# Unread products of a constant table between the steps of a threshold search (greedy routing of a mixture of experts)

## The chip, the cores and the metric

The program runs on one core of a Trainium2 chip. The metric is the device time of one execution in microseconds (us). The engines named here are TensorE (PE; PEld is its weight load), VectorE (DVE), ScalarE (ACT), GpSimd (POOL) and the DMA queues.

## The reference

Three layers follow one another on 20,224 tokens of 256 features: a gated recurrence, a mixture of 8 experts with greedy routing under a capacity, and a mixture of 8 experts with the best expert for each token. The change touches the routing of the second layer alone.

```python
# layer 1: h = f * h + (1 - f) * x, over 4 sequences of 5056 tokens, f from a sigmoid
# layer 2: greedy routing, cap = N // E = 2528 tokens to an expert
logits = x @ w_gate
order = np.argsort(-logits.flatten())
for idx in order:
    tok, e = (int(idx) // E, int(idx) % E)
    if assigned[tok] >= 0 or counts[e] >= cap:
        continue
    assigned[tok] = e
    counts[e] += 1
for e in range(E):
    mask = assigned == e
    out[mask] = np.maximum(x[mask] @ w1[e], 0.0) @ w2[e]
# layer 3: argmax expert for each token, result scaled by its softmax weight
```

## The kernel before

The kernel has six stages with a barrier between them: constants, the recurrence with the scores (`scan_stage`), greedy routing (`route_greedy`), the experts of layer 2, the routing of layer 3 and its experts.

Scores lie in a table of 128 partitions x 8 experts x 160 columns. Greedy routing is done in 7 phases (`PH`). In a phase each unassigned token bids for its best open expert (`bids`, lines 747 to 758, all on DVE), and a search finds the lowest threshold at which no expert overflows. A search round tests 16 thresholds at once. DVE compares all bids with them (`above`, line 787) in 4 pieces (`PIECES`). PE counts, for each expert and threshold, the bids above: 20 products of `choice` (64 wide weights) with 128 columns of `above`, 5 to a piece, added up in `cP` (line 681). DVE takes the diagonal and sums it (`part_cnt`, lines 794 and 796), PE sums over groups (`eP`, line 685), DVE compares with what each expert needs (`fills`, line 798), PE adds over experts (`aP`, line 687), and DVE counts (`nfill`, line 800) and makes the next thresholds (lines 805 and 808). Every step waits for the one before through a semaphore; only the pieces of `above` overlap with PE.

A phase has 3 rounds (`TRIED`) and then a test whether all bids above the low end fit (line 695). Only where they don't are 4 more rounds and an exact cut run. In these inputs one phase of seven does that, so there are 6 x 3 + 7 = 25 rounds.

After the last phase `place_rows` and `place_products` find for each slot of an expert the token that lies there. PE adds 160 products of 320 columns into `r_found_ps` (line 480), the first with start=True. That tensor isn't read before line 548, after all 160. `c.emin_full` is a constant bf16 table, 8 - e for expert e, made before the first stage.

Of the kernel before, what the change touches and what calls it, by code (L numbers as in the profile page):

```python
# [30 lines left out]
P = 128  # L31
# [47 lines left out]
def alone(eng, passed):  # L79

    eng.sem_inc(passed, 1)
# [357 lines left out]
def place(nc, ctx, m, cols):  # L439

    r = Consts()
    sb = lambda n, s, d=F32: ctx.enter_context(nc.sbuf_tensor(m + n, s, d))
    sem = lambda n: ctx.enter_context(nc.semaphore(m + n))
    r.cols = cols
    r.own = sb("own", [P, E])
    r.run = sb("run", [P, E, NG])
    r.shift = sb("shift", [P, E])
    r.mine = sb("mine", [P, E, NG])
    r.slot = sb("slot", [P, NG])
    r.slot_i = sb("slot_i", [P, 3, NG], I32)  # L450
    r.slot_b = sb("slot_b", [P, 2, NG], BF16)
    r.grid_col = sb("grid_col", [P, NG], BF16)


    r.hit_place = sb("hit_place", [P, 2, J // 2, P, 2], BF16)
    r.hit_tile = sb("hit_tile", [P, 2, J // 2, cols, 2], BF16)
    r.hit_row = sb("hit_row", [P, 2, J // 2, 2, cols, 2], BF16)
    r.found = sb("found", [P, 2, cols])
    r.base_ps = ctx.enter_context(nc.psum_tensor(m + "base_ps", [P, 2, E], F32))
    r.found_ps = ctx.enter_context(nc.psum_tensor(m + "found_ps", [P, 2, cols], F32))  # L460
    r.own_ready = sem("p_own_ready")
    r.base_ready = sem("p_base_ready")
    r.tile_ready = sem("p_tile_ready")
    r.part_ready = sem("p_part_ready")
    r.hits_ready = sem("p_hits_ready")
    r.hits_used = sem("p_hits_used")
    return r


def place_products(pe, c, r):  # L470

    pe.wait_ge(r.own_ready, 1)
    pe.matmul(r.base_ps[:, 0, :], c.tri[:], r.own[:], start=True, stop=True)
    pe.matmul(r.base_ps[:, 1, :], c.ones[:], r.own[:], start=True, stop=True).then_inc(r.base_ready, 1)

    def group(g, b, begin, end):
        pe.wait_ge(r.hits_ready, g + 1)
        pe.wait_ge(r.part_ready, g + 1)
        for j in range(J):
            mm = pe.matmul(r.found_ps[:], r.hit_place[:, b, j // 2, :, j % 2], r.hit_row[:, b, j // 2, :, :, j % 2],  # L480
                           start=(begin and j == 0), stop=(end and j == J - 1), skip_group_check=True)
        mm.then_inc(r.hits_used, 1)

    group(0, 0, True, False)
    group(1, 1, False, False)
    with pe.Fori(1, NG // J // 2 - 1) as g:
        group(2 * g, 0, False, False)
        group(2 * g + 1, 1, False, False)
    group(NG // J - 2, 0, False, False)
    group(NG // J - 1, 1, False, True)  # L490
# [60 lines left out]
def route_greedy(nc, c, w1, w2):  # L551
# [3 lines left out]
    with ExitStack() as ctx:  # L555
# [59 lines left out]
        r = place(nc, ctx, "r_", NG)  # L615
# [25 lines left out]
        @block.sync  # L641
        def _(sp):
            load_weights(sp, c, w1, w2, 0, raw)
# [13 lines left out]
        @block.tensor  # L657
        def _(pe):
            groups = NG // Q
            piece = groups // PIECES  # L660

            def columns(q):
                return choice[:, q, :, :].rearrange("p e n -> p (e n)")

            def count_mask(n, mask):

                pe.wait_ge(mask_ready, n + 1)
                for q in range(groups):
                    mm = pe.matmul(qP[:], columns(q), mask[:, q * Q:(q + 1) * Q], start=(q == 0), stop=(q == groups - 1))
                mm.then_inc(mask_counted, 1)  # L670

            def sum_mask(n):
                pe.wait_ge(mask_row_ready, n + 1)
                pe.matmul(nP[:], c.ones[0:E * Q, :], mask_row[:], start=True, stop=True).then_inc(mask_summed, 1)

            def count_round(n):
                for q in range(groups):
                    if q % piece == 0:
                        pe.wait_ge(above_ready, PIECES * n + 1 + q // piece)

                    mm = pe.matmul(cP[:].rearrange("m t q -> m (t q)"), columns(q),  # L681
                                   above[:, :, q * Q:(q + 1) * Q], start=(q == 0), stop=(q == groups - 1))
                mm.then_inc(counted, 1)
                pe.wait_ge(part_ready, n + 1)
                pe.matmul(eP[:], c.sel[:], part_cnt[:], start=True, stop=True).then_inc(summed, 1)
                pe.wait_ge(fills_ready, n + 1)
                pe.matmul(aP[:], c.ones_b[:], fills[0:E, :], start=True, stop=True).then_inc(filled, 1)

            with pe.Fori(0, PH) as k:
                pe.wait_ge(choice_ready, k + 1)  # L690
                alone(pe, passed)
                for n in range(TRIED):
                    count_round(k * ROUNDS + n)
                pe.wait_ge(try_ready, k + 1)
                pe.matmul(nP[:], c.ones[0:E, :], cnt_row[:], start=True, stop=True).then_inc(tried_summed, 1)
                pe.wait_ge(over_ready, k + 1)
                alone(pe, passed)
                over_now = pe.value_load(over[0:1, 0:1], min_val=0, max_val=1)
                with pe.If(over_now > 0):
                    for n in range(TRIED, ROUNDS):  # L700
                        count_round(k * ROUNDS + n)
                    count_mask(2 * k, sure)
                    sum_mask(2 * k)
                    pe.wait_ge(own_edge_ready, k + 1)
                    pe.matmul(oP[:], c.tri[:], own_edge[:], start=True, stop=True).then_inc(before, 1)
                    count_mask(2 * k + 1, taken)
                    sum_mask(2 * k + 1)
                with pe.If(over_now < 1):

                    for sem_of_round in (counted, summed, filled):  # L710
                        pe.sem_inc(sem_of_round, ROUNDS - TRIED)
                    pe.sem_inc(before, 1)
                    pe.sem_inc(mask_counted, 2)
                    pe.sem_inc(mask_summed, 2)
            place_products(pe, c, r)
# [992 lines left out]
```

## Time and profile before

| | us |
|---|---|
| median of 3 runs | 2828.97 |
| lowest, highest | 2825.3, 2830.41 |
| profiled execution, its own time | 2830.13 |
| span of its trace | 2828.4 |
| search, first and last product of `cP` (start) | 255.2, 522.6 |
| products of `r_found_ps` (start) | 554.3 to 595.3 |

PE is busy for 87% of the span, DVE for 45%. That is an average over stages: in the experts PE is the busy engine, in the search it is DVE, and PE's products are short stations of a chain between two DVE instructions. How to read the views: a wait names the instruction for which an engine sat idle, and a timeline row gives start, duration, instruction and the idle time before it in brackets.

### The profile page before, as it was taken

To read this page: it belongs to the slowest core of one execution; us is meant where nothing else is said; L and a number is where in the kernel's file an instruction comes from. 1 tells how busy PE (TensorE), PEld (TensorE's weight loads), DVE (VectorE), ACT (ScalarE), POOL (GpSimd) and SP (SyncE) were. 2 spreads that over 40 slices of the span, in tenths; PEclk is the share of its full clock that TensorE was granted. 3 is DMA by queue.
4 is the path that set the end of the run, shared out by engine and by line. 5 is a ranking of instruction groups with operands and counts; after the bars stand their busy time and mean duration, and the time that the engine had idled before them with its cause. 6 is when DMAs were issued, how large, how long until landed. Compare 5 with 4: busy or idle time off the path is not lost. (4 is left out here: it accounts for less than half of the span.)

```text
span 2828.4 us, 42796 instructions
## 1 busy us (share of the span) xinstructions
PE 2450.3 (87%) x14391; PEld 2092.6 (74%) x14392; DVE 1277.1 (45%) x2306; ACT 738.9 (26%) x1386; POOL 797.8 (28%) x765
## 2 busy tenths in 40 slices
PE   7992333269999999999999945999999999999998
PEld 6991222148888888888888832888888888888887
DVE  6776777863434343434433367333333333333332
ACT  3540000132222222222222214222222222222222
POOL 2332000031313131322311120435535443535332
PEclk9995555589999999999999978999999999999999
DMA  7991000021212121212111111212212121211111
GB/s 245 311 305 49 0 0 0 0 64 55 75 37 74 37 72 39 67 45 68 44 37 45 37 52 38 67 45 68 70 45 72 44 74 45 69 45 40 39 45 34
DMA packets 100823, 183.66 MB, mean 65 GB/s; under 512 B 12797, under 2 KB 70399, under 8 KB 100800
## 3 DMA queue, kind: packets, MB, share of 16 engines
q1 hardware_dynamic: 33328, 75.00, 8.2%
q0 software_dynamic: 24960, 66.02, 7.9%
q10 hardware_dynamic: 42512, 42.38, 4.3%
q8 instruction: 9, 0.15, 0.0%
q14 instruction: 14, 0.11, 0.0%
HBM read 120.26 MB, written 65.44 MB: 66 GB/s over the span
## 5 line engine op out<-in xcount | busy, mean ns | idle before, releaser
L1639 DVE SCALAR_TENSOR_TENSOR m_hl<-m_hP,m_hh 128x512 fp32r<-128x512 f32 x352 | 243.5, 692 | 664.4 <-ACT m_hh L1596 664.4
L1331 DVE SCALAR_TENSOR_TENSOR m_hl<-m_hP,m_hh 128x512 fp32r<-128x512 f32 x320 | 221.4, 692 | 581.3 <-ACT m_hh L1284 581.3
L1596 ACT ACTIVATE m_hh<-m_hP 128x512 fp32r<-128x512 f32 x352 | 210.5, 598 | 664.3 <-PE m_hP L1548 664.3
L1284 ACT ACTIVATE m_hh<-m_hP 128x512 fp32r<-128x512 f32 x320 | 191.1, 597 | 680.9 <-PE m_hP L1192 680.9
L1104 POOL COPY m_idx<-rows_i 128x4 int32 (+1 forms) x41 | 7.6, 185 | 1049.8 <-PE m_tP L1161 703.6
L681 PE MATMUL cP<-above,choice 128*64 128x128 bf16 x500 | 73.7, 314 | 156.0 <-DVE above L787 156.0
L1490 POOL DMA_INDIRECT m_xg<-y_rows,m_idx x180 | 173.8, 965 | 86.2 <-POOL m_idx L1486 39.3
L1501 POOL DMA_INDIRECT out_dram<-m_rows,m_dest x176 | 175.5, 997 | 69.6 <-issue 52.5
L681 PEld LDWEIGHTS cP<-above,choice 128*64 128x64 bf16 x500 | 50.1, 162 | 175.9 <-DVE above L787 175.9
L1108 POOL DMA_INDIRECT m_xg<-h_rows,m_idx x164 | 156.4, 954 | 74.1 <-issue 40.8
L1486 POOL COPY m_idx<-rows_i 128x4 int32 (+1 forms) x45 | 8.4, 187 | 526.4 <-PE m_tP L1538 459.6
L1559 PEld LDWEIGHTS m_yP<-w_1h,m_hh 128*128 128x128 f32 x704 | 103.9, 189 | 19.9 <-DVE m_hl L1639 9.8
L1559 PEld LDWEIGHTS m_yP<-w_0h,m_hh 128*128 128x128 f32 x704 | 103.9, 189 | 19.6 <-DVE m_hl L1639 9.5
L1559 PE MATMUL m_yP<-w_1h,m_hh 128*128 128x256 f32 x704 | 117.9, 290 | 0.2
L499 ACT ACTIVATE r_hit_row<-r_hit_tile,part 128x1280 bf16<-128x1280 bf16 x20 | 27.2, 1362 | 347.7 <-DVE r_hit_tile L535 347.7
L1559 PE MATMUL m_yP<-w_0h,m_hh 128*128 128x256 f32 x704 | 117.9, 290 | 0.2
L1548 PE MATMUL m_hP<-m_xh,w_0h 128*128 128x512 f32 x352 | 112.2, 400 | 2.2 <-DVE m_xl L1635 1.4
L1559 PE MATMUL m_yP<-w_1h,m_hl 128*128 128x256 f32 x704 | 113.0, 282 | 0.0
L1559 PE MATMUL m_yP<-w_0h,m_hl 128*128 128x256 f32 x704 | 112.9, 282 | 0.0
L1559 PE MATMUL m_yP<-w_0l,m_hh 128*128 128x256 f32 x704 | 112.1, 281 | 0.0
L1559 PE MATMUL m_yP<-w_1l,m_hh 128*128 128x256 f32 x704 | 112.1, 281 | 0.0
L1548 PE MATMUL m_hP<-m_xh,w_1h 128*128 128x512 f32 x352 | 111.4, 398 | 0.0
(300 smaller groups left out, 5582.7 us busy)
## 6 DMA issues: line engine op xcount, KB each, us to landing
w_raw<-in_moe_w_dram SPq DMA_DIRECT2D x32, 1024.0 KB, 6.9
y_rows<-m_rows ACTq DMA_DIRECT2D x41, 516.0 KB, 3.5
f_in<-in_f_logit_dram SPq DMA_DIRECT2D x39, 512.0 KB, 4.6
x_in<-in_x_dram SPq DMA_DIRECT2D x39, 512.0 KB, 6.9
h_rows<-rows ACTq DMA_DIRECT2D x39, 512.0 KB, 5.7
m_xg<-y_rows,m_idx POOLq DMA_INDIRECT x180
out_dram<-m_rows,m_dest POOLq DMA_INDIRECT x176
m_xg<-h_rows,m_idx POOLq DMA_INDIRECT x164, 2.8
```

The lines of the kernel that those rows point to most:

```text
L499: act.activation(r.hit_row[:, b, :, 0, :, :].rearrange("p g n j -> p g (n j)"), r.hit_tile[:, b, :, :, :].rearrange("p g n j -> p g (n j)" ...
L681: mm = pe.matmul(cP[:].rearrange("m t q -> m (t q)"), columns(q), above[:, :, q * Q:(q + 1) * Q], start=(q == 0), stop=(q == groups - 1))
L1108: pool.indirect_dma_start(xg[:, k, :], None, src[:, :], bass.IndirectOffsetOnAxis(ap=idx[:, k:k + 1].bitcast(U32), axis=0)).then_inc(gathe ...
L1284: act.activation(hh[f % 2][:], hP[f % 2][:], ACT.Relu).then_inc(hh_ready, 1)
L1331: dve.scalar_tensor_tensor(out=hl[f % 2][:], in0=hP[f % 2][:], scalar=0.0, in1=hh[f % 2][:].bitcast(F32), op0=ALU.max, op1=ALU.subtract).t ...
L1486: pool.tensor_copy(idx[:], c.rows_i[:, bass.ds(i * TPC, TPC)]).then_inc(idx_ready, 1)
L1490: pool.indirect_dma_start(xg[:, k, :], None, src[:, :], bass.IndirectOffsetOnAxis(ap=idx[:, k:k + 1].bitcast(U32), axis=0)).then_inc(gathe ...
L1501: pool.indirect_dma_start(dst[:, :], bass.IndirectOffsetOnAxis(ap=dest[:, k:k + 1].bitcast(U32), axis=0), rows[:, k, :], None, bounds_chec ...
L1548: mm = pe.matmul(hP[f % 2][:], c.w1_s[b][s][:, d, f * P:(f + 1) * P], x[:, d, :], start=(q == 0), stop=(q == len(terms) - 1))
L1559: mm = pe.matmul(yP[k][:, 0:D], h[f % 2][:, k * P:(k + 1) * P], c.w2_s[b][s][:, f, :], start=(f == 0 and q == 0), stop=(f == FC - 1 and q ...
L1596: act.activation(hh[f % 2][:], hP[f % 2][:], ACT.Relu).then_inc(hh_ready, 1)
L1639: dve.scalar_tensor_tensor(out=hl[f % 2][:], in0=hP[f % 2][:], scalar=0.0, in1=hh[f % 2][:].bitcast(F32), op0=ALU.max, op1=ALU.subtract).t ...
```

## The change

In `route_greedy` the PE program gets a helper that issues n products of `c.emin_full` into `r.found_ps` (128 wide weights, 320 columns, bf16). Each is a group of its own, and nobody reads it. The helper is called before the waits of pieces 2, 3 and 4, before the wait for `part_cnt`, before the wait for `fills`, and three times after `aP`: 8 products in each round, 200 in 25 rounds. No semaphore, no other engine and no other stage is touched.

```diff
+            def keep_going(n):
+
+                for _ in range(n):
+                    pe.matmul(r.found_ps[:], c.emin_full[:, 0, 0:P], c.emin_full[:, 0:2, :],
+                              start=True, stop=True, skip_group_check=True)
+
             def count_round(n):
                 for q in range(groups):
                     if q % piece == 0:
+                        if q:
+                            keep_going(1)
                         pe.wait_ge(above_ready, PIECES * n + 1 + q // piece)
 
                     mm = pe.matmul(cP[:].rearrange("m t q -> m (t q)"), columns(q),
                                    above[:, :, q * Q:(q + 1) * Q], start=(q == 0), stop=(q == groups - 1))
                 mm.then_inc(counted, 1)
+                keep_going(1)
                 pe.wait_ge(part_ready, n + 1)
                 pe.matmul(eP[:], c.sel[:], part_cnt[:], start=True, stop=True).then_inc(summed, 1)
+                keep_going(1)
                 pe.wait_ge(fills_ready, n + 1)
                 pe.matmul(aP[:], c.ones_b[:], fills[0:E, :], start=True, stop=True).then_inc(filled, 1)
+                keep_going(3)
```

On PE, in the loop over phases, the end of a search round stands like this before (the last two pieces, the two sums, and the first piece of the next round):

```order
L681 MATMUL cP<-above,choice 64x128 [waits r_above_ready]
L681 MATMUL cP<-above,choice 64x128 x4
L679 REGISTER_ALU
L681 MATMUL cP<-above,choice 64x128 [waits r_above_ready]
L681 MATMUL cP<-above,choice 64x128 x4
L684 REGISTER_ALU
L685 MATMUL eP<-part_cnt,sel 128x16 [waits r_part_ready]
L687 MATMUL aP<-fills,ones_b 128x16 [waits r_fills_ready]
L679 ISA
L681 MATMUL cP<-above,choice 64x128 [waits r_above_ready]
```

The same place on PE after the change:

```order
L689 MATMUL cP<-above,choice 64x128 x4
L679 MATMUL r_found_ps<-emin_full 128x320
L687 REGISTER_ALU
L689 MATMUL cP<-above,choice 64x128 [waits r_above_ready]
L689 MATMUL cP<-above,choice 64x128 x4
L679 MATMUL r_found_ps<-emin_full 128x320
L693 REGISTER_ALU
L694 MATMUL eP<-part_cnt,sel 128x16 [waits r_part_ready]
L679 MATMUL r_found_ps<-emin_full 128x320
L697 MATMUL aP<-fills,ones_b 128x16 [waits r_fills_ready]
L679 MATMUL r_found_ps<-emin_full 128x320 x3
L687 ISA
```

Every added product stands ahead of the product that waits, never behind it, and the order of the others is as it was.

## Rows read from the trace of the kernel before

**Rows 1.** The page: span, and the granted clock in 40 slices.

```profile
span 2828.4 us, 42796 instructions
...
PEclk9995555589999999999999978999999999999999
```

**Rows 2.** Who waited for whom, 255 to 538 us: total, times, longest.

```profile
PE cP L681 <- DVE above L787: 156.0, 25, 36.2
...
DVE part_q L794 <- PE cP L681: 17.5, 25, 0.8
DVE fills L798 <- PE eP L685: 17.4, 25, 0.7
...
DVE any_fills L800 <- PE aP L687: 7.1, 25, 0.3
```

**Rows 3.** Timeline around one round: start, duration, instruction, idle time before.

```profile
506.95 2.95 PE L681 MATMUL cP<-above,choice 128*64 128x128 bf16 x20 [14.75 <-DVE above L787]
...
509.94 0.28 DVE L794 TENSOR_TENSOR part_q<-cP,diag 64x128 f32<-64x128 f32 x1 [0.36 <-PE cP L681]
...
512.60 3.03 DVE L787 TENSOR_TENSOR above<-bid,thr 128x640 bf16<-128x640 f32 x4
...
513.48 2.95 PE L681 MATMUL cP<-above,choice 128*64 128x128 bf16 x20 [1.77 <-DVE above L787]
514.21 0.50 PEld L681 LDWEIGHTS cP<-above,choice 128*64 128x64 bf16 x5 [0.24 <-DVE above L787]
...
515.68 0.50 PEld L681 LDWEIGHTS cP<-above,choice 128*64 128x64 bf16 x5 [0.23 <-DVE above L787]
516.46 0.28 DVE L794 TENSOR_TENSOR part_q<-cP,diag 64x128 f32<-64x128 f32 x1 [0.83 <-PE cP L681]
...
517.11 0.60 PE L685 MATMUL eP<-part_cnt,sel 64*128 64x16 f32 x2 [0.69 <-DVE part_cnt L796]
...
518.04 0.19 PE L687 MATMUL aP<-fills,ones_b 8*128 8x16 bf16 x1 [0.33 <-DVE fills L798]
...
519.12 3.03 DVE L787 TENSOR_TENSOR above<-bid,thr 128x640 bf16<-128x640 f32 x4
```

**Rows 4.** Timeline, PE alone, 554 to 557.5 us.

```profile
554.26 3.55 PE L480 MATMUL r_found_ps<-r_hit_row,r_hit_place 128*128 128x320 bf16 x13 [11.04 <-ACT r_hit_row L499]
```

**Rows 5.** Timeline, PE alone, 558.5 to 577 us.

```profile
561.16 1.29 PE L480 MATMUL r_found_ps<-r_hit_row,r_hit_place 128*128 128x320 bf16 x8 [0.71 <-ACT r_hit_row L499]
563.31 1.29 PE L480 MATMUL r_found_ps<-r_hit_row,r_hit_place 128*128 128x320 bf16 x8 [0.86 <-ACT r_hit_row L499]
```

**Rows 6.** Line 480, 552 to 557.5 us: durations ns (min, median, max).

```profile
L480 PEld LDWEIGHTS r_found_ps<-r_hit_row,r_hit_place x14: 103/144/145, 554.2 to 557.4; 128*128 128x128 bf16 x14
L480 PE MATMUL r_found_ps<-r_hit_row,r_hit_place x13: 396/468/469, 554.3 to 557.4; 128*128 128x320 bf16 x13
```

**Rows 7.** Line 480, 560 to 594 us.

```profile
L480 PE MATMUL r_found_ps<-r_hit_row,r_hit_place x132: 300/302/305, 559.7 to 593.3; 128*128 128x320 bf16 x132
```

**Rows 8.** Line 681.

```profile
L681 PE MATMUL cP<-above,choice x500: 310/314/317, 255.2 to 522.6; 128*64 128x128 bf16 x167
```

**Rows 9.** Line 685.

```profile
L685 PE MATMUL eP<-part_cnt,sel x50: 370/380/394, 258.9 to 523.9; 64*128 64x16 f32 x50
```

**Rows 10.** Line 1181, 700 to 1600 us.

```profile
L1181 PE MATMUL m_sP<-m_wg,m_yT x550: 175/256/257, 699.8 to 1584.5; 128*128 128x8 f32 x184
```

**Rows 11.** Busy time of each engine by stretch, then granted clock, DMA.

```profile
255.00:538.00 283.00, 101.92 (x635) 72.19 (x635) 209.73 (x549) 0.00 (x0) 0.00 (x0) 0.50 0.00 0
563.00:595.00 32.00, 19.99 (x125) 11.11 (x126) 31.12 (x46) 20.60 (x16) 0.00 (x0) 1.00 0.00 0
164.00:168.00 4.00, 3.35 (x30) 3.03 (x28) 3.22 (x6) 1.69 (x4) 1.86 (x2) 1.00 0.93 316
168.00:169.00 1.00, 1.00 (x9) 1.00 (x8) 1.00 (x2) 0.60 (x1) 0.00 (x0) 0.74 1.08 371
```

**Rows 12.** Timeline, PE alone, 164 to 173 us.

```profile
165.09 1.85 PE L259 MATMUL sP<-wg,h 128*128 128x8 f32 x16
167.54 0.65 PE L237 MATMUL fP<-ident,f_in 128*128 128x128 f32 x4 [0.60 <-DMA x_in<-in_x_dram]
```

## The prediction

> **What bounds the kernel now.** I read the page first for the clock by slices: TensorE is granted half speed (1.2 GHz) in the slices of the greedy search and full speed (2.4 GHz) nearly everywhere else [rows 1]. The table by stretch says the same for 255 to 538 us: clock 0.50, PE busy 102 of 283 us, DVE 210 [rows 11]. So the search belongs to DVE, and PE matters only where DVE waits for it. The waits give these: 17.5 us for `cP`, 17.4 for `eP`, 7.1 for `aP`, in 25 rounds each, 42 us of the search in all [rows 2]. All else in a round is DVE's own work. The timeline of one round shows the stations, from `above` at 512.60 to the next at 519.12, 6.52 us: DVE waits 0.83, 0.70 and 0.28 us [rows 2, 3]. PE also waits: 1.77 us ahead of the first piece, 0.69 and 0.33 ahead of the sums, and 14.75 us ahead of a phase, while DVE makes the bids [rows 3]. The added products go into these gaps, except the long one.
>
> The change can act in two ways only: through time that an added product takes from one that DVE waits for, and through the granted clock.
>
> **The price of an added product at 1.2 GHz.** The same shape (320 columns, 128 wide weights) runs in line 480. In the stretch at 1.2 GHz 13 of them take 3.55 us, the last 0.47, so they start every (3.55 - 0.47)/12 = 0.26 us [rows 4, 6]; at 2.4 GHz 8 take 1.29, one 0.30, so every 0.141 us [rows 5, 7].
>
> Between pieces: pieces start every (515.68 - 513.48)/3 = 0.733 us, as DVE delivers them [rows 3]. The last one runs from 515.68 to 516.43 (513.48 + 2.95), 0.75 us for five products of 0.314, so one starts every (0.75 - 0.314)/4 = 0.109 us [rows 3, 8]. A piece then occupies PE for 0.545 us, and with an added product for 0.81, which is 0.07 to 0.08 more than DVE's pace. Three insertions push the last piece back by 0.22 us, and DVE waits for it. 25 rounds: 5.5 us. At 2.4 GHz a piece takes 5 x 0.056 + 0.141 = 0.42 us and nothing is late.
>
> The other five cost nothing. The one behind `cP` ends 0.3 us into a gap of 0.69; the one behind `eP` has 0.33 us of gap for 0.26, and its results drain beside the wait; the three behind `aP` need 0.8 of 1.77 us [rows 3]. If the middle one didn't fit, `aP` would be at most 0.14 us late. The three ahead of the overflow test end before it, since DVE has four small instructions to do first. Queue and semaphores are as before. `r_found_ps` is written first for real with start=True, after a long DVE stretch.
>
> Weights: the filler has 128 wide ones, and those of `choice` come back behind it. In line 480 each product loads such weights (0.144 us) and they still start every 0.26 us, so they are hidden [rows 4, 6]. I take nothing for them; the other bound is one load of 0.144 exposed at each insertion, 3 x 25 x 0.144 = 10.8 us.
>
> The Trainium skill, TensorE: Matmul & The Clock Gate, section "The mechanism" of Part 3, speaks against the change: a weight load overlaps products in flight only where it goes to other rows of the array. By that rule both swaps would show, and twice the bound above would be added. The row of 13 products at a pace of 0.26 us doesn't bear it out.
>
> **What the clock would give.** At 2.4 GHz the last piece ends earlier by 4 x (0.109 - 0.056) plus some 0.09 on the last product (320 columns: 0.468 against 0.302, of which the columns are 0.12), 0.30 us. `eP` is two products, 0.60 us together; a product of the same kind with 8 columns takes 0.256 at 2.4 GHz against 0.380, so 0.60 x 0.256/0.380 = 0.40, 0.20 us less [rows 3, 9, 10]. `aP`, 0.19, loses perhaps 0.03. Sum 0.53 us for a round that is wholly at 2.4 GHz, and it doesn't pay the 0.22. Even the first round of a phase, where DVE waits only 0.36 us for `cP` because it has other work, can take the 0.30 [rows 3]. Upper bound of the change: 25 x 0.53 = 13.3 us.
>
> **Does the clock rise, and where.** Set the density of each stretch beside its clock. The search before streams 20 x 128 = 2,560 columns in 6.52 us, 390 a us, and stays at 1.2 GHz throughout [rows 3, 11]. Line 480 started from a long idle time, streamed without a gap at 1.2 GHz, and was at 2.4 GHz soon after 557.5 us; it stays there at 8 x 320 columns every 2.15 us, 1,190 a us [rows 4, 5, 11]. After the change a round has two halves. From the first piece to the end of the filler behind `cP` PE streams 3,840 columns in some 3.2 us (1.2 GHz: nearly without a gap, like line 480). The rest, some 3.5 us, has four fillers and two small sums, 1,280 columns, under 400 a us: as thin as the search before. The nearest row at 2.4 GHz for a thin stretch lies in the recurrence: PE looks busy for 3.35 of 4 us at 164 to 168, but much of it is 16 products of 8 columns (165.09) and then 0.60 us of idle time; right behind it the clock falls (0.74 in 168 to 169) [rows 11, 12]. So I expect that the dense half raises the clock in part of the rounds, and that the thin half loses it before the next dense one: the clock is up where little is to be gained. Where it rises near the end of the dense half, `eP` and `aP` become 0.23 us shorter, sometimes with a part of the last piece. I take 0.25 us in 10 of 25 rounds, between none and all by nothing better than the split of the round: 2.5 us back.
>
> Sum: 5.5 - 2.5 = 3.0 us. The profiled execution took 2830.13 (1.2 above the median of the three runs), so 2833.1 in its terms and 2832.0 against the median. All differences below 0.2% (5.7 us) can't be told from none by a measurement of this kernel.
>
> **The rivals.**
> - The clock holds at 2.4 GHz from the first burst of a phase to its last round. For it: PE's gaps within a round shrink to under 1 us, and line 480 holds 2.4 GHz while PE is busy for 20 of 32 us [rows 11]. Against it: the thin half. Time: the first round of each phase stays slow (7 x 0.22 = 1.5 us), 18 others gain 0.53 (9.5): -8 us, 2821.
> - The skill's page on TensorE, section "Why this matters for your kernels", ties the fall to idle gaps between bursts alone. By it this rival would win. The fall at 168 us, behind a gap of 0.60 us, speaks against it.
> - Slower: the weight swaps show. At an insertion one load of 0.144 us comes on top, each piece starts 0.22 instead of 0.07 us late, and the end of `cP` moves by 0.66 us a round: +16.4 - 2.5 = +13.9, 2843. For it: `cP` changes from 64 to 128 wide weights and back, which no row shows. Against it: the pace of line 480. It decides from 0.036 us exposed at an insertion (2.7 us over 75 of them, on top of 3.0).
> - The clock never rises: +5.5, 2834.5, within my forecast's range.
> - Between the first two: 2.4 GHz is held through some phases, by how they fall; -5 to 0 us.
>
> **How the numbers follow.** Forecast (with the clock never up) 0.52, clock held 0.22, weight swaps 0.14, in between 0.12. The likeliest time is 2832.0, its own range 2829 to 2836. To leave out no more than 2 in 10 the range takes in most of the held clock (to 2820) and the lighter part of the exposed loads (to 2839). Faster by over 0.2%: most of the held clock, 0.19. Slower: the swaps and the edge of the forecast, 0.19. The same: 0.62.
>
> **What would show it.** In the trace after: the granted clock alternates between 0.50 and 1.00 in the search; the pieces of `cP` start 0.8 us apart in rounds at 1.2 GHz, 0.73 in those at 2.4; DVE's wait for `cP` grows from 17.5 us towards 20 and those for `eP` and `aP` shrink by 1 to 3 us in all. I am wrong if the clock is 1.00 through whole phases (DVE's three waits then lose 8 us or more), or if the pieces start over 0.85 us apart. The placing of tokens, the experts and the time outside 255 to 538 us stay as they are.

## The result and the profile after

| | before | after |
|---|---|---|
| median of 6 runs, us | 2826.59 | 2849.32 |
| lowest to highest | 2825.08 to 2830.41 | 2843.87 to 2853.62 |
| ratio | | 1.0075 (1.0065 to 1.0085) |
| profiled execution, span | 2828.4 | 2845.8 |

The kernel became slower by 0.75%, 21 us (18 to 24; the two medians lie 22.7 us apart). The forecast was 2832.0, with a range from 2820 to 2839.

The page after, where the clock by slices reads as before [rows 1]:

```profile
span 2845.8 us, 43196 instructions
...
PEclk9995555589999999999999978999999999999999
```

The waits around the search, 249 to 545 us (total, times, longest), to be read beside [rows 2]:

```profile
PE cP L689 <- DVE above L798: 141.4, 25, 34.8
DVE part_q L805 <- PE cP L689: 40.7, 25, 1.8
...
DVE fills L809 <- PE eP L694: 15.9, 25, 0.7
...
DVE any_fills L811 <- PE aP L697: 7.0, 25, 0.3
```

DVE waits 40.7 us for `cP` where it waited 17.5; for `eP` 15.9 instead of 17.4 and for `aP` 7.0 instead of 7.1. The sum is 63.6 against 42.0: 21.6 us more, which is as much as the result. The span of this execution is only 17.4 us longer because its recurrence, which runs ahead of the changed code, ended some 5 us sooner than in the execution before (the first product of the search starts at 250.3 instead of 255.2).

The timeline of PE for one round at 1.2 GHz (start, duration, instruction, idle time before), to be read beside [rows 3]:

```profile
520.73 0.74 PE L689 MATMUL cP<-above,choice 128*64 128x128 bf16 x5 [14.76 <-DVE above L798]
521.41 0.45 PE L679 MATMUL r_found_ps<-emin_full 128*128 128x320 bf16 x1
521.78 0.74 PE L689 MATMUL cP<-above,choice 128*64 128x128 bf16 x5
...
525.32 0.60 PE L694 MATMUL eP<-part_cnt,sel 64*128 64x16 f32 x2 [0.31 <-DVE part_cnt L807]
525.86 0.45 PE L679 MATMUL r_found_ps<-emin_full 128*128 128x320 bf16 x1
526.25 0.19 PE L697 MATMUL aP<-fills,ones_b 8*128 8x16 bf16 x1
526.38 0.98 PE L679 MATMUL r_found_ps<-emin_full 128*128 128x320 bf16 x3
528.22 0.74 PE L689 MATMUL cP<-above,choice 128*64 128x128 bf16 x5 [0.86 <-DVE above L798]
```

Pieces start 1.05 us apart (520.73, 521.78), not 0.733 as before and not 0.81 as forecast. The filler starts 0.68 us after its piece, though five products at 0.109 occupy 0.545, and the next piece starts 0.37 us after the filler, though 320 columns occupy 0.26. So 0.13 us is lost ahead of the filler and 0.11 behind it, and no semaphore is named for either.

The clock did in kind what was forecast. Busy time by stretch, then the granted clock:

```profile
415.00:421.00 6.00, 5.14 (x28) 2.70 (x27) 3.95 (x9) 0.00 (x0) 0.00 (x0) 0.50 0.00 0
422.00:424.00 2.00, 1.10 (x7) 0.47 (x6) 1.41 (x6) 0.00 (x0) 0.00 (x0) 1.00 0.00 0
425.00:428.00 3.00, 3.00 (x18) 1.71 (x17) 1.60 (x3) 0.00 (x0) 0.00 (x0) 0.50 0.00 0
```

The dense half of a round (to 421) runs at 1.2 GHz, the thin one (422 to 424) at 2.4, and the next dense one at 1.2 again. In the whole search 7 such stretches had the full clock, 24 us together. In the thin stretch `eP` is down to 0.39 us:

```profile
421.78 0.39 PE L694 MATMUL eP<-part_cnt,sel 64*128 64x16 f32 x2 [0.30 <-DVE part_cnt L807]
```

### The profile page after: what moved, and what is told of

Its sections match the earlier page's. It is cut to its first block and busy times, and to the rows that moved or that the text cites. A ratio compares the mean times of both kernels' runs of the same rounds, so it can differ in the third digit from the quotient of the medians.

```text
span 2845.8 us, 43196 instructions
## 1 busy us (share of the span) xinstructions
PE 2504.4 (88%) x14591; PEld 2104.0 (74%) x14592; DVE 1277.2 (45%) x2306; ACT 738.3 (26%) x1386; POOL 798.8 (28%) x765
## 5 line engine op out<-in xcount | busy, mean ns | idle before, releaser
L1119 POOL DMA_INDIRECT m_xg<-h_rows,m_idx x164 | 156.4, 954 | 74.1 <-issue 40.7
L1559 PE MATMUL m_hP<-m_xl,w_0h 128*128 128x512 f32 x352 | 111.3, 398 | 0.0
```

Source lines behind the costliest of these rows:

```text
L1119: pool.indirect_dma_start(xg[:, k, :], None, src[:, :], bass.IndirectOffsetOnAxis(ap=idx[:, k:k + 1].bitcast(U32), axis=0)).then_inc(gathe ...
L1559: mm = pe.matmul(hP[f % 2][:], c.w1_s[b][s][:, d, f * P:(f + 1) * P], x[:, d, :], start=(q == 0), stop=(q == len(terms) - 1))
```

## The experiments

All times are against the kernel before on the same chip in the same session. The chips differed: before had a median of 2875.96 us beside the first four kernels, 2830.87 beside the next four, and 2830.09 beside the last two. Only differences are compared. A round's length is read from the starts of `above` on DVE in each trace.

### Fillers as wide as their neighbours (e1_narrow)

```diff
-                    pe.matmul(r.found_ps[:], c.emin_full[:, 0, 0:P], c.emin_full[:, 0:2, :],
+                    pe.matmul(r.found_ps[0:E * Q], c.emin_full[:, 0, 0:E * Q], c.emin_full[:, 0:2, :],
```

> The fillers get 64 wide weights, as cP has, and write 64 partitions; columns, number and places stay. Theory W (the trace after shows pieces 1.055 us apart where 0.545 + 0.267 were expected: 0.24 us is lost at each insertion because the weights change between 64 and 128 wide, and such a load does not overlap the product in flight): pieces at 1.2 GHz start 0.81 us apart, a round takes 6.75 instead of 7.48 us, time +1 to +5 us against before. Rival S (any foreign product loses this time, by its other PSUM bank, its own start, or the semaphore of the load behind it): pieces stay 1.05 us apart, time +19 to +24 us.

The edit is against the kernel after. Measured: ratio 1.0004 (0.9995 to 1.0013), +1 us. A round at 1.2 GHz takes 6.73 us. PE's timeline of the first two pieces of a round:

```profile
508.99 0.74 PE L689 MATMUL cP<-above,choice 128*64 128x128 bf16 x5 [14.76 <-DVE above L798]
509.53 0.47 PE L679 MATMUL r_found_ps<-emin_full 128*64 128x320 bf16 x1
509.79 0.74 PE L689 MATMUL cP<-above,choice 128*64 128x128 bf16 x5
```

The filler starts 0.54 us after its piece and the next piece 0.26 after the filler: both pauses are gone and 0.80 is left, as the columns alone give. Same place, same columns, same tensor, same semaphores; only the width of the weights (and with it the partitions of the output) is another. S is out. Width of weights and partitions of the output change together in all runs here, so they aren't told apart.

The weight loads show where the time goes. After the change, the load of the first filler and that of the piece behind it:

```profile
521.40 0.10 PEld L679 LDWEIGHTS r_found_ps<-emin_full 128*128 128x128 bf16 x1 [0.17 <-issue]
...
521.78 0.50 PEld L689 LDWEIGHTS cP<-above,choice 128*64 128x64 bf16 x5 [0.28 <-issue]
```

The same two with 64 wide fillers:

```profile
509.42 0.18 PEld L679 LDWEIGHTS r_found_ps<-emin_full 128*64 128x64 bf16 x1
...
509.73 0.56 PEld L689 LDWEIGHTS cP<-above,choice 128*64 128x64 bf16 x5
```

With equal widths a load starts 0.11 and 0.06 us ahead of its product (509.53, 509.79), while the product before still runs. With unequal widths it starts with its product (521.41, 521.78), and the idle time before it has no releaser but "issue".

The time of this kernel isn't a measure of the width alone: its rounds at 1.2 GHz are 0.75 us shorter than after (7.48), 19 us in 25 rounds, and its search is at full clock for 41 us instead of 24. The added columns cost it some 5 us (25 x 0.20), of which the clock gives most back.

### No fillers between the pieces (e2_none_between)

```diff
-                        if q:
-                            keep_going(1)
```

> The three fillers between the pieces of a round are left out, the five others stay. If all the loss is at the insertions between pieces, a round takes 6.53 us or less, and the time is that of before or 0 to 3 us less (the clock may still rise in some rounds). If the fillers behind cP, eP and aP cost something too (the middle one stands in the shortest gap), the time is above before by up to 25 x 0.14 = 3.5 us.

The edit is against the kernel after. Measured: ratio 0.9999 (0.9990 to 1.0009), no difference. Rounds take 6.53 us, the clock stays at 1.2 GHz, and the waits are those of [rows 2]:

```profile
DVE part_q L803 <- PE cP L687: 17.5, 25, 0.8
DVE fills L807 <- PE eP L692: 17.5, 25, 0.7
```

The five fillers behind `cP`, `eP` and `aP` cost nothing that shows in DVE's waits, though they are 128 wide as well: what a change of width takes there falls into PE's own waits.

### Only the fillers between the pieces (e3_only_between)

```diff
                 mm.then_inc(counted, 1)
-                keep_going(1)
...
-                keep_going(1)
...
-                keep_going(3)
```

> Only the three fillers between the pieces stay (128 wide weights). If the loss is there, rounds at 1.2 GHz take 6.53 + 3 x 0.32 = 7.48 us, the clock rises in fewer rounds since five fillers are gone, and the time is +20 to +24 us. If the loss is made by the sum of all fillers (the queue, instruction fetch), it falls to 3/8 of it, +8 us.

The edit is against the kernel after. Measured: ratio 1.0085 (1.0071 to 1.0098), +24 us. Rounds at 1.2 GHz take 7.48 us, as after. The three fillers between the pieces make the whole loss. The five others in the kernel after gave back at most the difference to its +21 us, which the two intervals don't tell from nothing; in the traces its search is at full clock for 24 us, this one's for 14.

### The swap without the columns (e4_thin, e5_thin96, e9_thin64)

Three fillers in a round, between pieces, of 32 columns only, with 128, 96 and 64 wide weights; the edit is against e3_only_between. e5_thin96 and e9_thin64 ran once each and are read from their traces, not from their times.

```diff
-                    pe.matmul(r.found_ps[:], c.emin_full[:, 0, 0:P], c.emin_full[:, 0:2, :],
+                    pe.matmul(r.found_ps[:, 0, 0:32], c.emin_full[:, 0, 0:P], c.emin_full[:, 0, 0:32],
```

The other two have `r.found_ps[0:96, ...]` with `0:96` and `r.found_ps[0:64, ...]` with `0:64`.

> As the kernel with fillers only between the pieces, but of 32 columns instead of 320, with the same 128 wide weights. Theory W: a piece then takes 0.545 + 0.03 + 0.24 = 0.81 us, pieces start 0.81 apart, the last is 0.24 late, +6 us. If the loss comes from the columns (a product of 320 columns that takes longer beside DVE or in this bank) a piece takes 0.57, less than DVE's 0.733, and nothing is late: 0.

> The thin filler (32 columns, three in a round, between pieces) with 96 wide instead of 128 wide weights; cP keeps 64. If any change of width costs (theory W), pieces at 1.2 GHz start 0.81 us apart and a round takes 6.77, as with 128. If only the full 128 wide load is special (its faster kind of load), pieces start 0.735 apart, a round takes 6.53. Read from the trace, not from the time.

> Control for the thin fillers: 32 columns, three in a round between pieces, now with the 64 wide weights that cP has. Theory W (a change of width drains the array): a piece takes 0.545 + 0.03, pieces start 0.735 us apart, a round takes 6.53. If any foreign product between cP's costs: 0.81 and 6.77, as with 128 wide weights. Read from the trace.

PE's timeline from one piece to the next, 128 wide:

```profile
516.31 0.74 PE L689 MATMUL cP<-above,choice 128*64 128x128 bf16 x5 [1.77 <-DVE above L795]
516.98 0.21 PE L679 MATMUL r_found_ps<-emin_full 128*128 128x32 bf16 x1
517.12 0.74 PE L689 MATMUL cP<-above,choice 128*64 128x128 bf16 x5
```

96 wide:

```profile
515.63 0.74 PE L689 MATMUL cP<-above,choice 128*64 128x128 bf16 x5 [14.76 <-DVE above L795]
516.30 0.26 PE L679 MATMUL r_found_ps<-emin_full 128*96 128x32 bf16 x1
516.50 0.74 PE L689 MATMUL cP<-above,choice 128*64 128x128 bf16 x5
```

64 wide:

```profile
517.77 0.74 PE L689 MATMUL cP<-above,choice 128*64 128x128 bf16 x5 [1.77 <-DVE above L795]
518.31 0.23 PE L679 MATMUL r_found_ps<-emin_full 128*64 128x32 bf16 x1
518.51 0.74 PE L689 MATMUL cP<-above,choice 128*64 128x128 bf16 x5
```

| weights of the filler | piece to piece, us | round, us |
|---|---|---|
| 128 wide | 0.81 | 6.77 |
| 96 wide | 0.87 | 6.92 |
| 64 wide, like `cP` | 0.74 (DVE's pace) | 6.53 |

With 128 wide weights the time was 1.0025 (1.0016 to 1.0034), +7 us. The filler of 64 wide weights starts 0.54 us behind its piece, the two others 0.67. With 96 wide weights I had said 0.81 or 0.735; it is 0.87, so a change of width costs there too, and 0.05 us more than with 128. So the loss isn't a property of the full width but of the change, as far as fillers wider than their neighbours show it; a narrower one was not tried.

Why 96 is dearer stands in the weight loads. The filler's load, 128 wide:

```profile
516.98 0.10 PEld L679 LDWEIGHTS r_found_ps<-emin_full 128*128 128x128 bf16 x1 [0.17 <-issue]
```

96 wide:

```profile
516.30 0.16 PEld L679 LDWEIGHTS r_found_ps<-emin_full 128*96 128x96 bf16 x1 [0.17 <-issue]
```

The 96 wide load takes 0.06 us longer. Both fillers start 0.67 us behind their piece, and it is behind the filler that 96 loses: the next piece starts 0.20 us after it, not 0.14. So the part of the loss behind the filler fits the filler's own load, which nothing hides: 0.10 of the 0.11 us with 128 wide weights. The 0.13 us ahead of it are the same for both.

### Fillers sized to the gaps (e6_dense)

The edit is against the kernel after. Weights 64 wide; 1 x 192 columns between pieces, 3 x 300 behind `cP`, 1 x 300 behind `eP`, 6 x 320 behind `aP`.

```diff
+            def keep_going(n, cols=320):
+                table = c.emin_full[:].rearrange("p e n -> p (e n)")
+                spare = r.found_ps[0:E * Q].rearrange("p a n -> p (a n)")
+                for _ in range(n):
+                    pe.matmul(spare[:, 0:cols], table[:, 0:E * Q], table[:, 0:cols],
+                              start=True, stop=True, skip_group_check=True)
...
-                            keep_going(1)
+                            keep_going(1, 192)
...
-                keep_going(1)
+                keep_going(3, 300)
...
-                keep_going(1)
+                keep_going(1, 300)
...
-                keep_going(3)
+                keep_going(6)
```

> Fillers with 64 wide weights, sized to fit each gap at 1.2 GHz (1 of 192 columns between pieces, 3 of 300 behind cP, 1 of 300 behind eP, 6 of 320 behind aP). Nothing is late at 1.2 GHz, and a round has some 6,200 columns. If density is what was missing, the clock rises in the first round of a phase and holds to its last: 18 of 25 rounds take about 6.0 us instead of 6.53, time -7 to -10 us. If the clock still falls in every round: -1 to -4. If more fillers cost by themselves (queue, instruction fetch): above 0.

Measured: ratio 0.9975 (0.9963 to 0.9987), 7 us faster than before (4 to 10). DVE's three waits sum to 32.9 us in its trace, 9.1 less than before. Clock by stretch (the rounds of the first phase, the bids behind them, and the whole search):

```profile
255.00:275.00 20.00, 14.06 (x110) 9.39 (x110) 15.20 (x44) 0.00 (x0) 0.00 (x0) 0.91 0.00 0
275.00:288.00 13.00, 0.00 (x0) 0.00 (x0) 9.59 (x21) 0.00 (x0) 0.00 (x0) 0.52 0.01 3
...
255.00:514.00 259.00, 124.19 (x943) 83.47 (x944) 198.82 (x517) 0.00 (x0) 0.00 (x0) 0.74 0.00 0
```

A later round at the full clock, DVE's waits for PE:

```profile
437.60 3.03 DVE L800 TENSOR_TENSOR above<-bid,thr 128x640 bf16<-128x640 f32 x4
441.19 0.28 DVE L807 TENSOR_TENSOR part_q<-cP,diag 64x128 f32<-64x128 f32 x1 [0.56 <-PE cP L691]
...
442.27 0.23 DVE L811 TENSOR_SCALAR fills<-eP,need_p 128x16 bf16<-128x16 f32 x1 [0.48 <-PE eP L696]
442.78 0.17 DVE L813 TENSOR_SCALAR_CACHE_REDUCE any_fills<-aP 128x16 f32<-128x16 f32 x1 [0.27 <-PE aP L699]
...
443.63 3.03 DVE L800 TENSOR_TENSOR above<-bid,thr 128x640 bf16<-128x640 f32 x4
```

The round takes 6.03 us (437.60 to 443.63) instead of 6.52. DVE waits 0.56, 0.48 and 0.27 us, against 0.83, 0.70 and 0.28 [rows 2, 3]. The clock is lost in every stretch of bids (0.52) and comes back in the first round or after it, so first rounds take 6.3 to 6.5 us.

### Fillers through the bids as well (e7_through_bids, e8_wide_bids)

```diff
+            def during_bids(k):
+                for step, n, cols in ((2, 5, 300), (3, 3, 300), (4, 1, 320), (5, 1, 320), (6, 5, 300), (7, 3, 300),
+                                      (8, 1, 320), (9, 1, 320), (10, 1, 240), (11, 3, 300), (12, 4, 320)):
+                    pe.wait_ge(dv, SETUP + k * PHASE + step)
+                    keep_going(n, cols)
```

and 4 fillers each before the wait for the test and at the end of the phase without overflow. e8_wide_bids is the same with 128 wide weights.

> As the dense kernel, and fillers also beside each of DVE's steps of the bids (PE waits for the step before, then issues what fits) and around the test at the end of a phase. If the clock is held from phase to phase, all 25 rounds take 6.0 us: -11 to -14 us. If it's lost in the 3 us around the test alone: first rounds a little slower, -9 to -12. Rival: DVE's steps of the bids slow down beside PE's reads, or PE comes late into a phase: a gain smaller than that of the dense kernel.

> As the kernel with fillers through the bids, but with 128 wide weights. Theory W prices a swap at 0.11 to 0.13 us at 1.2 GHz and about 0.09 at 2.4, so at a held 2.4 GHz a piece with its filler takes 0.28 + 0.08 + 0.2 = 0.56 us, less than DVE's 0.733, and the width costs nothing: within 2 us of the 64 wide kernel. If the clock is at 1.2 when a phase begins, its first round takes 7 us or more. If the width costs time also at 2.4 GHz: +5 or more against the 64 wide kernel.

Measured: 64 wide 0.9972 (0.9961 to 0.9984), not to be told from e6_dense (0.9975); 128 wide 1.0010 (1.0002 to 1.0019). The first expectation failed. The fillers didn't hold the clock through a phase (the search as a whole, and the bids of one phase, 64 wide weights):

```profile
255.00:520.00 265.00, 188.10 (x1147) 113.40 (x1148) 202.67 (x522) 0.00 (x0) 2.86 (x1) 0.74 0.00 0
280.00:294.00 14.00, 8.76 (x34) 3.70 (x32) 10.23 (x25) 0.00 (x0) 0.00 (x0) 0.76 0.01 2
```

The mean clock of the search is 0.74, the same as without fillers in the bids, and rounds of 6.54 and 6.03 us follow one another. What the clock wins in the bids, where DVE waits for no product, it loses within the rounds: DVE's three waits sum to 35.0 us, against 32.9 in e6_dense. Why is open. The trace is that of the slowest of the six executions (2829.57 us, median 2823.38), whose search began 5.5 us later than that of e6_dense, so it stands for the clock and the rounds, not for the time.

The second failed as well in its main number (11 us above the 64 wide kernel, not within 2), since the clock wasn't held there either, but its two kinds of round answer the question. At 1.2 GHz a round takes 7.28 us. At 2.4 GHz one takes 6.03, as with 64 wide weights (starts of `above`):

```profile
296.99 3.03 DVE L812 TENSOR_TENSOR above<-bid,thr 128x640 bf16<-128x640 f32 x4
...
303.02 3.03 DVE L812 TENSOR_TENSOR above<-bid,thr 128x640 bf16<-128x640 f32 x4
```

PE in that round:

```profile
297.87 0.47 PE L692 MATMUL cP<-above,choice 128*64 128x128 bf16 x5 [0.85 <-DVE above L812]
298.27 0.26 PE L682 MATMUL r_found_ps<-emin_full 128*128 128x192 bf16 x1
298.60 0.47 PE L692 MATMUL cP<-above,choice 128*64 128x128 bf16 x5
```

Here the filler starts 0.40 us behind its piece (0.30 in e6_dense, 438.48 to 438.78), so the swap still costs 0.10, but the piece with it fits into DVE's 0.733. In this kernel the width is paid only where the clock is low.

### The dense tail alone (e10_dense_tail)

```diff
-                        if q:
-                            keep_going(1, 192)
```

> The dense kernel without its fillers between the pieces; the ten behind cP, eP and aP stay. cP's own 2,560 columns are then all that PE streams in that half of a round. If the tail's fillers are enough to hold 2.4 GHz once it is there, the time is that of the dense kernel, -6 to -9 us. If the first half is then too thin, the clock falls within rounds and little is left: -1 to -4 us.

The edit is against e6_dense. Measured: ratio 0.9981 (0.9972 to 0.9990), 5 us faster, between the two expectations. The search as a whole:

```profile
255.00:514.00 259.00, 134.10 (x850) 85.47 (x850) 196.87 (x515) 0.00 (x0) 0.00 (x0) 0.65 0.00 0
```

The mean clock is 0.65 against 0.74 with the three fillers between pieces. More rounds stay at 6.53 us, but those that are at full clock take 6.03 or 6.04. DVE's three waits sum to 35.1 us, 2.2 more than in e6_dense. The difference between the two kernels (0.0006) is within their intervals.

## Why the prediction was wrong

- **What bounds the search**: right. The whole difference is in DVE's three waits for PE; in the experts and the layer behind, the last 2,220 us of the kernel, PE is busy as long as before (2130 and 2129 us) at the same clock, 0.98.
- **The lag of the pieces**: the step that failed. I counted the columns alone, took the weights as hidden, and got 0.22 us a round. The change of width adds 0.24 us at each of three insertions, and the pieces start 1.05 us apart, beyond the 0.85 that I had named as the sign of being wrong: a round at 1.2 GHz takes 7.48 us instead of 6.53. 3 x (1.05 - 0.735) = 0.95 us, over 25 rounds 23.6; the clock gives some 2 us back and 21.6 remain. The columns' part was right: with 64 wide weights a round takes 6.73, 0.20 more.
- **Why the row misled me**: 13 products in a row each loaded new 128 wide weights at a pace of 0.26 us [rows 4]. That shows that loads hide behind products of the same width. It says nothing of a 128 wide load behind a 64 wide product, and I put the one for the other although I wrote that no row shows the change. The bound that I gave (one load of 0.144 exposed, 10.8 us) was too small too: neither the filler's load nor that of the piece behind it runs ahead, and an insertion loses 0.24 us, 75 x 0.24 = 18 us. The bound should have been two loads, 21.6 us. That 0.24 is near two loads doesn't make it two loads: the rows show 0.13 ahead of the filler's load and 0.11 behind, and what the engine does in the 0.13 is not shown.
- **The rule that I set aside**: by the Trainium skill (TensorE: Matmul & The Clock Gate, "The mechanism" in Part 3) a load overlaps products in flight only where it goes to other rows of the array. The same section also excepts a load that goes to a background buffer, which I left out. The rule called for a slower kernel, and the kernel is slower; with twice my bound, as I had worked it out, my sum would have been 24.6 us for the 21 measured. As I quoted it, it isn't borne out: in e1_narrow weights of one width on the same 128 rows are loaded 0.11 us ahead of their product, and in e1_narrow and e9_thin64 the filler follows its piece without a pause. What the runs show is a cost for a change of width.
- **The fillers behind `cP`, `eP` and `aP`**: right, they cost nothing (e2_none_between).
- **What the clock gives**: right. `eP` 0.39 us at 2.4 GHz (0.40 forecast), a wholly fast round 6.03 (6.52 - 0.53 = 5.99 forecast).
- **Where the clock rises**: right in kind. 7 short stretches, mostly in the thin half, 24 us in all, and no phase at full clock. By the sum above it is worth about 2 us (2.5 forecast). The rounds say the same: from the first `above` to the last the search takes 285.4 us instead of 264.8, 20.6 more, where 24 rounds wholly at 1.2 GHz would make it 22.8.
- **The rivals**: "the weight swaps show" was the right one in kind, with a chance of 0.14 and +13.9 us; the measured loss lies beyond it. It deserved the bigger chance, since the forecast rested on one row for another shape. Against the held clock I had set the fall behind a gap of 0.60 us at 168. In the same trace TensorE sits idle for 0.60 us before 81.71 too, and the clock stays at 1.00 from 76 to 86 us, so such a gap alone decides nothing.

## What to carry to other kernels

A product that nobody reads is free only if it fits into the wait at the slow clock, with the cost of a change of width counted in (0.24 us an insertion here). So size it from the pace of the engine that is waited for, and where the wait is short take the columns of its weights from the product beside it. Filling the gaps of the whole round paid here: 7 us in e6_dense. With a thin stretch behind each dense one, in the kernel after, the clock is up where little is to be gained. More filling is no sure gain: with fillers in the bids as well (e7_through_bids) the time was the same, and why the clock fell within rounds is open. A row that shows a cost as hidden holds for its own sequence of shapes, so bound a mixed sequence by both loads exposed.

## What the runs showed of the hardware

- A 128 wide product between 64 wide ones costs TensorE 0.13 us ahead of it and 0.11 behind at 1.2 GHz (0.10 ahead of it at 2.4). With 96 wide weights it costs 0.05 us more, as much as its load is longer (0.15 to 0.16 us against 0.10). Between products of 64 wide weights there is no pause, also where the output tensor changes (e1_narrow).
- Whether a change of rows costs anything is open. `aP` has 8 rows and the fillers behind it 128, both 128 wide. The filler starts 0.13 us behind `aP` (526.25 to 526.38 in the timeline after), which is far more than 16 columns occupy at the pace of the others (some 0.013 us, an estimate from 320 columns in 0.26). So up to 0.12 us are lost there too, next to a product too short to hide a load of 0.10.
- The fillers left DVE's own steps as they were: the four pieces of `above` take 3.03 us beside them too, as in [rows 3].
